# Attention steps that run two and three steps behind their scores, in a fused RWKV, expert and gated-MLP kernel

## The reference

```python
logits = x @ w_gate                      # 4 experts, the best 2 of each token count
for e in range(E):
    q = x @ wq[e]; k = x @ wk[e]; v = x @ wv[e]
    scores = scale * (q @ k.transpose(0, 2, 1))
    scores = np.where(causal, -1000000000.0, scores)
    scores = scores - scores.max(-1, keepdims=True)
    a = np.exp(scores)
    a /= a.sum(-1, keepdims=True) + 1e-09
    ye = a @ v @ wo[e]
    ...                                  # out += gate of (token, e) * ye
h = np.maximum(x @ w_in, 0.0)
u, v = (h[..., :d_ff // 2], h[..., d_ff // 2:])
...                                      # v_n = v, normalised over its features
v_s = np.einsum('ts,bsd->btd', w_spatial, v_n) + b_spatial[None, :, None]
return ((u * v_s) @ w_out).astype(np.float32)
```

## Time and profile before

| what | us |
|---|---|
| median of 3 runs (lowest to highest) | 1192.07 (1189.08 to 1203.58) |
| profiled execution | 1204.56 |
| its span, first to last instruction | 1202.8 |
| TensorE busy over the span | 1023.1 (85%) |
| VectorE, ScalarE, GpSimd busy | 513.3, 449.6, 257.7 |
| recurrence, from the span's start | to about 575 |
| attention steps of periods 0, 1, 2, 3 | 609 to 693, 740 to 832, 889 to 980, 1036 to 1128 |

### The profile page before, as it was taken

One profiled execution on the slowest core, in us unless ns is written; L12 is line 12 of the kernel. 1 busy time (PEld: TensorE's weight loads), 2 busy tenths in 40 slices (PEclk: granted clock), 3 DMA queues, 4 the chain that ended last, 5 costly groups with the idle time before them and its releaser, 6 DMA issues.

```text
span 1202.8 us, 36880 instructions
## 1 busy us (share of the span) xinstructions
PE 1023.1 (85%) x15696; PEld 733.9 (61%) x15696; DVE 513.3 (43%) x1423; ACT 449.6 (37%) x1112; POOL 257.7 (21%) x355
## 2 busy tenths in 40 slices
PE   1699889898898898986677699987999879998989
PEld 1677777787777777875533465444654455544545
DVE  4567666575676665642232234231233313332120
ACT  1455544454454454621133332332323323233400
POOL 7354435344343343310100000100001000010011
PEclk9889999998999988986798899998999989999989
DMA  2322423323234242211800000001000010000000
GB/s 83 106 63 75 130 73 91 111 74 112 87 89 114 74 123 76 73 49 30 259 11 2 1 1 0 1 6 60 1 1 1 6 61 1 1 1 11 23 0 33
DMA packets 50644, 63.49 MB, mean 53 GB/s; under 512 B 26545, under 2 KB 36593, under 8 KB 50481
## 3 DMA queue, kind: packets, MB, share of 16 engines
q1 hardware_dynamic: 50480, 61.13, 17.4%
HBM read 53.22 MB, written 7.86 MB: 51 GB/s over the span
## 4 chain that ended last, share of the span: by engine, by line
PE 40%; ACT 6%; DVE 2%; DMA 2%; issue 1%; SPq 0%
PE banks L1344 9%; PE banks L1230 5%; PE banks L1249 4%; PE banks L1281 4%; ACT probs L1176 4%; PE banks L1269 4%; PE banks L1311 3%; PE banks L1298 3%; PE banks L1216 3%; PE banks L1356 2%; ACT probs_t L1119 2%; DVE probs L1440 2%; DMA x_tok<-x_dram 1%; PE banks L1201 1%; PE banks L1325 1%
## 5 line engine op out<-in xcount | busy, mean ns | idle before, releaser
L366 ACT ACTIVATE powers_z<-powers,parity 128x256 f32<-128x256 f32 x240 | 108.7, 501 | 213.6 <-DVE powers L757 211.7
L1114 POOL TENSOR_TENSOR v_st<-v_st,u_t 128x384 f32<-128x384 f32 x32 | 31.9, 997 | 577.1 <-DVE v_st L1498 577.1
L1344 PE MATMUL banks<-w_st,v_n 128*128 128x384 f32 x384 | 150.7, 509 | 4.9 <-issue 4.9
L335 POOL TENSOR_TENSOR state<-state_sum,dc 128x160 f32<-128x160 f32 x92 | 68.3, 743 | 303.2 <-DVE state_sum L865 303.2
L1176 ACT ACTIVATE probs<-probs,neg_max 128x128 f32<-128x128 f32 (+5 forms) x96 | 63.4, 660 | 174.6 <-DVE neg_max L1440 174.6
L512 PE MATMUL banks<-pq,powers_z 64*64 64x64 f32 (+1 forms) x3072 | 118.6, 230 | 9.9 <-issue 6.8
L512 PEld LDWEIGHTS banks<-pq,powers_z 64*64 64x64 f32 x3072 | 107.9, 144 | 13.1 <-issue 10.4
L1440 DVE CUSTOM_DVE_ANT_0 probs<-banks,hide 128x128 f32<-128x128 f32 (+5 forms) x96 | 56.0, 622 | 91.7 <-PE banks L1249 91.4
L857 DVE SCALAR_TENSOR_TENSOR vu_tok<-banks,minus,vz_tok 128x80 f32<-128x80 f32 x192 | 48.9, 297 | 105.3 <-PE banks L688 105.2
L1344 PEld LDWEIGHTS banks<-w_st,v_n 128*128 128x128 f32 x384 | 65.3, 193 | 43.4 <-issue 17.9
L1269 PE MATMUL banks<-ident,probs 128*128 128x128 f32 x336 | 55.4, 282 | 42.1 <-ACT probs_t L1119 40.6
(11 more groups left out here) (156 smaller groups left out, 1845.7 us busy)
## 6 DMA issues: line engine op xcount, KB each, us to landing
w_ch<-decays_dram SPq DMA_DIRECT2D x48, 160.0 KB
kb_raw<-kb_ch_dram SPq DMA_DIRECT2D x48, 160.0 KB
vz_tok<-vz_tok_dram SPq DMA_DIRECT2D x24, 320.0 KB, 4.5
rz_ch<-rz_ch_dram SPq DMA_DIRECT2D x48, 160.0 KB
x_dram<-y_tok SPq DMA_DIRECT2D x384, 10.0 KB, 1.5
a_raw<-a_ch_dram SPq DMA_DIRECT2D x48, 80.0 KB
vc_tok<-vc_tok_dram SPq DMA_DIRECT2D x24, 160.0 KB, 5.2
r_ch<-r_ch_dram SPq DMA_DIRECT2D x48, 80.0 KB
```

Source lines behind the costliest of these rows:

```text
L335: pool.tensor_tensor(state[:, d % 2], state_sum[:, :, :], dc[:, v % 4, d].unsqueeze(2).to_broadcast([P, Q, D]), ALU.mult)\
L366: act.activation(powers_z[:, i, :, j, :], powers[:, i, :, :], ACT.Copy, scale=parity[:, j:j + 1])\
L1344: ins = pe.matmul(bank[M_BANK + j % 2][:, 0:TH], v_n[:, i, d * P:d * P + P], w_st[:, i, t], start=(i == 0), stop=(i == BLOCKS - 1))
```

## The change

Three things, in the code of all engines:

1. Attention work is turned two passes behind its scores and multiplied with the values three passes behind; `probs` gets a third buffer, and the loop has one pass more (s = 0 to 14). Shares and scaling move by one pass too.
2. On ScalarE a pass is copy of piece 0, exponential of expert 0, copy of piece 1, exponential of expert 1, further copies.
3. SP's loop loads x[n + 1] right after x[n] is transposed, before it waits for outputs of sequence n - 1.

Besides, one slot (-1, 0) is put ahead of the first scores of each period.

```diff
-        probs = sb("probs", [P, 2, 2, S])
+        probs = sb("probs", [P, 3, 2, S])
...
-        for s in range(STEPS + 2):
-            if 1 <= s <= STEPS:
-                blocks = 2 * ((s - 1) // EP + 1)
+        for s in range(STEPS + 3):
+            if 2 <= s < STEPS + 2:
+                blocks = 2 * ((s - 2) // EP + 1)
                 pieces += [(s, "probs", j, min(4, blocks - j)) for j in range(0, blocks, 4)]
-            if s >= 3 and s % EP == 1:
-                pieces.append((s, "share", (s - 3) // EP, EP))
+            if s >= 4 and s % EP == 0:
+                pieces.append((s, "share", (s - 4) // EP, EP))
...
-        slots = [(s, k) for s in range(STEPS + 2) for k in range(len(pieces_of(s)) + 2)]
+        slots = [(-1, 0)] + [(s, k) for s in range(STEPS + 3) for k in range(len(pieces_of(s)) + 2)]
...
-            for n in range(1, B + 1):
-                if n < B:
-                    sp.wait_ge(x_turned, at(n - 1, x_turned, BLOCKS))
-                    sp.dma_start(x_tok[:, :, :], x_dram[n].rearrange("(i p) f -> p i f", p=P)).then_inc(x_loaded, 16)
-                for i in range(BLOCKS):
-                    sp.wait_ge(y_read, at(n - 1, y_read, i + 1))
-                    sp.dma_start(out_dram[n - 1, i * P:i * P + P, :], out_tok[:, i, :]).then_inc(y_stored, 16)
+            for n in range(B + 1):
+                if n + 1 < B:
+                    sp.wait_ge(x_turned, at(n, x_turned, BLOCKS))
+                    sp.dma_start(x_tok[:, :, :], x_dram[n + 1].rearrange("(i p) f -> p i f", p=P)).then_inc(x_loaded, 16)
+                if n > 0:
+                    for i in range(BLOCKS):
+                        sp.wait_ge(y_read, at(n - 1, y_read, i + 1))
+                        sp.dma_start(out_dram[n - 1, i * P:i * P + P, :], out_tok[:, i, :]).then_inc(y_stored, 16)
...
-                    for s in range(STEPS + 2):
-                        if s < STEPS:
-                            i, p = s // EP, s % EP
-                            width = (i + 1) * P
-                            for a in range(2):
-                                e = 2 * p + a
-                                act.wait_ge(s_read, at(n, s_read, 2 * s + a + 1))
-                                act.activation(probs[:, s % 2, a, 0:width], probs[:, s % 2, a, 0:width], ACT.Exp,
-                                               scale=-1.0, bias=neg_max[:, i, e:e + 1], accum_out=den[:, i, e:e + 1])\
-                                    .then_inc(probs_ready, 1)
+                    outputs(n, 0, dense_upto(n, -1, 0))
+                    for s in range(STEPS + 3):
                         outputs(n, dense_from(n, s, 0), dense_upto(n, s, 0))
-                        for k, piece in enumerate(pieces_of(s)):
-                            turned(n, piece)
-                            outputs(n, dense_from(n, s, k + 1), dense_upto(n, s, k + 1))
                         last = len(pieces_of(s)) + 1
-                        outputs(n, dense_from(n, s, last), dense_upto(n, s, last))
+                        for k in range(max(2, last)):
+                            if k + 1 < last:
+                                turned(n, pieces_of(s)[k])
+                            if k < 2 and s < STEPS:
+                                exponentials(n, s, k)
+                            if k + 1 <= last:
+                                outputs(n, dense_from(n, s, k + 1), dense_upto(n, s, k + 1))
...
@@ turn, on TensorE
-                    pe.wait_ge(probs_ready, at(n, probs_ready, 2 * s))
+                    pe.wait_ge(probs_ready, at(n, probs_ready, 2 * (s - 1)))
...
-                        if s >= 2:
-                            times_v(n, s - 2)
+                        if s >= 3:
+                            times_v(n, s - 3)
...
@@ maxima, on VectorE
-                if s >= 2:
-                    dve.wait_ge(p_turned, at(n, p_turned, probs_upto(s - 1)))
+                if s >= 3:
+                    dve.wait_ge(p_turned, at(n, p_turned, probs_upto(s - 3)))
```

More of the change, by code:

```diff
@@ L1030, in probs_upto @@
         def probs_upto(s):
-            return max(m for m, piece in enumerate(pieces) if piece[0] <= s and piece[1] == "probs") + 1
+            return max(m for m, piece in enumerate(pieces) if piece[0] <= s + 2 and piece[1] == "probs") + 1
         def share_upto(i):
@@ L1124, in turned, with exponentials @@
                 act.wait_ge(p_turned, at(n, p_turned, m + 1))
-                dst = probs_t[:, (s - 1) % 2, j:j + k, :] if what == "probs" else share_t[:, j % 2, :, :]
+                dst = probs_t[:, s % 2, j:j + k, :] if what == "probs" else share_t[:, j % 2, :, :]
                 copy(dst.rearrange("p j t -> p (j t)"), bank[T_BANK][:, 0:k * P]).then_inc(p_read, 1)
+            def exponentials(n, s, a):
+                i, e = s // EP, 2 * (s % EP) + a
+                width = (i + 1) * P
+                act.wait_ge(s_read, at(n, s_read, 2 * s + a + 1))
+                act.activation(probs[:, s % 3, a, 0:width], probs[:, s % 3, a, 0:width], ACT.Exp, scale=-1.0,
+                               bias=neg_max[:, i, e:e + 1], accum_out=den[:, i, e:e + 1]).then_inc(probs_ready, 1)
             def outputs(n, lo, hi):
@@ L1261, in turn @@
                     pe.wait_ge(p_read, at(n, p_read, m))
-                width = (s - 1) // EP + 1
+                width = (s - 2) // EP + 1
                 for x in range(k):
@@ L1265, in turn @@
                         a, c = (j + x) // width, (j + x) % width
-                        src = probs[:, (s - 1) % 2, a, c * P:c * P + P]
+                        src = probs[:, (s - 2) % 3, a, c * P:c * P + P]
                     else:
@@ L1276, in times_v @@
                     pe.wait_ge(o_read, at(n, o_read, i))
-                pe.wait_ge(p_read, at(n, p_read, probs_upto(s + 1)))
+                pe.wait_ge(p_read, at(n, p_read, probs_upto(s)))
                 for j in range(i + 1):
@@ L1378, in _ @@
                     queries_and_keys(n)
-                    for s in range(STEPS + 2):
+                    slot(n, -1, 0)
+                    for s in range(STEPS + 3):
                         if s < STEPS:
@@ L1439, in maxima @@
                     both = banks[:, first:2 * a + 2, :].rearrange("p b t -> p (b t)")
-                    dve.tensor_tensor_reduce(out=probs[:, s % 2, a, 0:width], in0=both[:, 0:width],
+                    dve.tensor_tensor_reduce(out=probs[:, s % 3, a, 0:width], in0=both[:, 0:width],
                                              in1=hide[:, S - width:S], scale=-1.0, scalar=3e38,
@@ L1530, in _ @@
                             .then_inc(k_read, 1)
-                    for s in range(STEPS + 2):
+                    spatial(n, 0, dense_upto(n, -1, 0))
+                    for s in range(STEPS + 3):
                         if s < STEPS:
                             maxima(n, s)
-                        if s >= 2 and s % EP == 0:
-                            shares(n, s // EP - 1)
+                        if s >= 3 and s % EP == 1:
+                            shares(n, (s - 3) // EP)
                         last = len(pieces_of(s)) + 1
                         spatial(n, dense_from(n, s, 0), dense_upto(n, s, last))
-                        if s >= 3 and s % EP == 1:
-                            scaled_o(n, (s - 3) // EP)
+                        if s >= 4 and s % EP == 0:
+                            scaled_o(n, (s - 4) // EP)
                 else:
```

## The result

The changed kernel takes 1136.76 us in the median of 4 runs (1124.39 to 1142.88), the one before 1193.73 us in 4 runs; the ratio is 0.948, with an interval of 0.937 to 0.958. The ratios here are of the fast executions alone, which leaves out the one of 1142.88 us; the medians of all runs give 0.952. The forecast was 1143.6 in a range of 1130 to 1162. Later, in the last experiment, it was 1135.9 against 1193.3 us, ratio 0.949 (0.943 to 0.955).

A forecast was written before the change was run, and what follows sets the result against it. TensorE's work and its waits, for ScalarE's copies and the load of x, were taken as the bound. 17.0 + 14.1 + 17.4 = 48.5 us off the median of 1192.07 gave 1143.6 us, range 1130 to 1162.

The forecast's parts named there:

- Part 1, the load: Second and third period boundaries: x loaded early no longer holds TensorE, making them like the first; gain 17.0 us.
- Part 2: Attention steps of periods 1 to 3: shorter TensorE waits for ScalarE's copy and the key copy; gain 14.1 us.
- the sum 0.94 + 0.60 + 0.1 = 1.64 us: ScalarE's exponential, copy and signalling, from a copy's end until the next piece may be transposed; leaves waits of 0.9 to 1.0.
- the early slot: Slot ahead of the first scores: one dense matmul fills the 0.7 us wait for the key copy in periods 1 to 3.
- Part 3: Attention steps of period 0: shorter copy waits, 11.4 us, plus a higher clock, 6; gain 17.4 us, bounds 8 and 24.
- The 14 gaps: Pieces of period 0 behind an earlier piece of the same step with no fold matmul between: 0.85 us idle each, 12 together.
- the clock: TensorE in period 0's steps: work at 1.2 GHz costs 10 us; 6 taken as gain, bounds 0 and 10.
- the long waits: TensorE's five longest waits in 625 to 684, 1.99 to 3.03 us, each followed by a clock fall; shorter ones by none.
- The rule of the Trainium skill: Transposes don't count as matmul activity, so period 0's clock stays low; 1149.6 us; low-clock rival's chance 0.27.
- The interleaving gives back what it takes: Rival: exponential between copies makes the single transpose bank the bound; only load and key wait gain, 19 us, 1173; chance 0.07.
- Slower: Rival: maximum, exponential and copy in series per piece, 2.7 us x 44, giving 1247; decides from 1.5 us a piece; chance 0.02.
- The fifteenth pass: Extra pass of the attention loop: has no work of its own, only lengthens the tail by what is missing in front.

The follow-up runs named there:

- the last experiment: The changed kernel and its version with period 0's fold matmuls only in gaps between pieces, both run again: 1135.9 and 1127.2 us.
- e2: Changed kernel with SP's old loop, so without the early load of x: 1154.1 us, ratio 0.965 to the kernel before.
- e1: Kernel before with only SP's new loop, the early load of x: 1183.2 us, ratio 0.988 to the kernel before.
- e4: Changed kernel with both exponentials ahead of the copies on ScalarE: 1173.3 us, ratio 0.978 to the kernel before.
- e3: Kernel before with only ScalarE alternating copy and exponential: 1159.5 us, ratio 0.968 to the kernel before.
- e5: Changed kernel without the slot (-1, 0) ahead of the first scores: 1143.4 us in a single run.
- e7: Kernel before with alternating copies and exponentials, early load and early slot, but its old lag and two buffers: 1138.6 us, ratio 0.957 to the kernel before.
- e8: Changed kernel with both exponentials between the first and the second copy: 1136.4 us in a single run.
- e6: Changed kernel with the 12 fold matmuls of period 0 only in gaps between two pieces of one pass: 1123.7 us, ratio 0.942 to the kernel before.
- r2: Second run of the changed kernel with period 0's fold matmuls only in gaps between pieces: 1127.2 us, ratio 0.942 to the kernel before.

## Why the prediction was right, and where it was off

**Part 1, the load: right.** 17.0 forecast, 17.95 measured, and 17.9 for the load alone. I had taken the first boundary (10.2 us) as the model for the other two, and they came out at 9.75: half a microsecond less each, of which 0.33 is a short wait of the first one for an x copy that they do not have.

**Part 2: right in kind, too small.** 14.1 forecast, 21.1 measured. The step that failed is the sum 0.94 + 0.60 + 0.1 = 1.64 us from copy to copy. It counted ScalarE's rows as if they followed one another without overlap, and a signal on top. Measured is 0.49 + 0.92 = 1.41, so one exponential between two copies delays nothing here, and 1.0 us of waits stayed in a period and not 3.0. The trace of before had the number: on ScalarE a copy of 0.57 us starts at 814.30, the next one at 814.78, 0.48 later. The Trainium skill has it too ("ScalarE: Activation LUTs", What ACT_TABLE_LOAD costs): instructions of this kind that follow one another overlap by about 93 ns; the rows give 0.09 (0.57 - 0.48) to 0.11 us (0.60 - 0.49). The second term that was too small is the early slot, 0.7 forecast, while taking it out cost 1.8. The two do not simply add: of the 7.05 us of a period 6.0 are waits for the copy (7.0 to 1.0) and 0.7 the wait for the keys.

**Part 3: right in kind, too small.** 17.4 forecast, 22.3 measured. The 14 gaps were counted rightly (14 waits), each 0.78 and not 0.85; with 0.4 for a maximum at the start, 24.4 became 11.3, 13.1 us instead of 11.4. The other 9 us are, by subtraction, mostly the clock, of which I had taken 6 within my bound of 10. The 61.6 us lie just below the 62 to 68 that I had named as the sign of being right.

**The clock.** Of the steps of period 0, 28 single microseconds were below full clock before and 4 after. My reason, that the clock falls only behind the long waits, was wrong. (The fall that I put at 667.6 belongs at 667.2, by the mean of 0.60 over that microsecond in the earlier trace rows: behind the wait of 3.03 us, but inside the 0.78 that followed.) Here are the microseconds of the one fall that is left (TensorE's busy time, then the clock):

```profile
624.00:625.00 1.00, 0.27 (x3) 1.00 0.00 0
625.00:626.00 1.00, 0.63 (x4) 1.00 0.00 0
626.00:627.00 1.00, 0.41 (x2) 1.00 0.00 0
627.00:628.00 1.00, 0.35 (x3) 1.00 0.00 0
628.00:629.00 1.00, 1.00 (x3) 0.52 0.09 16
...
631.00:632.00 1.00, 1.00 (x8) 0.77 0.00 0
```

No wait there is over 0.78 us; the engine was busy for 0.27, 0.63, 0.41 and 0.35 of four microseconds, with three such waits in a row (they end at 625.05, 626.46 and 627.65), and then the clock was 1.2 GHz from 628 to about 631.5. So a fall can come behind a run of short waits too. It does not have to: e2 has the same three waits in its pass 10 and no fall. The number of such microseconds goes with the waits for the copy in period 0 only roughly: 28, 31 and 28 with 23 to 26 us of waits (before, e1, e4), 9 with 12 (e3), 4 or none with 11 to 14 (changed twice, e2, e5, e7, e8), none with 3.7 (e6, r2).

The rule of the Trainium skill ("TensorE: Matmul & The Clock Gate", Part 4, on transposes), used as a rival, gave 1149.6 us with the falls staying. The number of transposes is the same, and 24 of the 28 microseconds went: as a forecast for this kernel it failed. It is not refuted as a statement, since the four microseconds before the remaining fall held hardly anything but transposes. No run here tells that from plain idleness.

**The rivals.** "The interleaving gives back what it takes" fell with e3 and e8: the bank does set the pace at 1.41 us a piece, but the exponential fits inside it. "Slower" needed 1.5 us a piece and got none. The fifteenth pass cost nothing that shows: with fourteen passes (e7) a period takes 122.4 us and not less than 121.9.

**Median against profile.** I took the gain off the median and not off the profiled execution, and that was needed: the recurrence, not the steps, makes executions differ. Of the 61 us of stages, 57 show in the medians. The missing 4 us are within what the runs spread by, and I leave them open. They also flatter the forecast. The sum of the parts was short by 12.5 us (48.5 against 61.0), a fifth of the gain; that the time came out only 6.8 below 1143.6 is in part luck, since these 4 us and 1.7 of a higher median before went the other way.

## What to carry to other kernels

When a matmul engine waits for a copy, look at what stands in front of that copy in the copying engine's own queue before adding buffers or lag: putting it ahead of them gave 34 of 43 us, the extra lag with its third buffer about 5. Then put small independent matmuls exactly into the gaps that the one bank leaves, not evenly over the loop: that was worth another 10 us and kept the clock up. A load whose only condition is met early should not sit behind waits on other things in the same queue.

## What was new about the hardware here

- ScalarE starts the next instruction before the row of the one ahead ends: 0.49 us after the start of a 128x512 copy whose row says 0.60, and 0.92 to 0.94 after a 128x768 exponential, its accumulator read included. Sums along that queue have to be taken from start to start.
- The granted clock fell to 1.2 GHz behind three waits of 0.78 us in a row in the changed kernel, and did not behind the same three in e2. With those gaps filled (e6 and r2, 51.6 us of steps) it stayed at 1.00.
- The first 575 us, untouched by any of the kernels, end up to 19 us apart from one execution to the next, with a mean clock from 25 us on of 0.93 in the slowest (before) and 0.99 in the fastest (changed). Up to about their first x transposes TensorE was busy for 469 of 550 us in the one and 449 of 530 in the other. It was idle for 81 us in both, so the difference goes with the clock and not with waits.
